# One block for attention and routing, with the weight fold laid out anew between logits, counts and lists

## The reference, cut to what matters

```python
for t in range(S):                                   # attention, r, k, v: (4, 8, 768, 48)
    cur = einsum('bhd,bhe->bhde', u * k_t, v_t)
    y[:, :, t] = einsum('bhd,bhde->bhe', r_t, state + cur)
    state = w * state + einsum('bhd,bhe->bhde', k_t, v_t)
...
do_compute = x @ w_skip > 0                          # experts, x: (3072, 384)
logits = xc @ w_gate; e_idx = argmax(logits, 1)      # w_gate: (384, 8)
gate_w = softmax(logits)[e_idx]
out = xc + gate_w * (relu(xc @ w1[e]) @ w2[e])       # w1: (8, 384, 1024), w2: (8, 1024, 384)
...
h = (x @ w1) * (x @ w2) @ w3                         # gated layers, w1, w2: (384, 1024), w3: (1024, 1024)
return h @ w_out                                     # w_out: (1024, 384)
```

## Time and profile before

| | us |
|---|---|
| median of 3 runs (lowest, highest) | 625.05 (624.2, 626.12) |
| profiled execution, its own time | 628.02 |
| its span | 626.2 |
| PE busy, sum over the span | 607.0 |
| DVE, ACT, POOL busy | 294.6, 225.7, 149.3 |

### The profile page before, as it was taken

One profiled execution on the slowest core, in us unless ns is written; L12 is line 12 of the kernel. 1 busy time (PEld: TensorE's weight loads), 2 busy tenths in 40 slices (PEclk: granted clock), 3 DMA queues, 4 the chain that ended last, 5 costly groups with the idle time before them and its releaser, 6 DMA issues. The chain is left out here.

```text
span 626.2 us, 17333 instructions
## 1 busy us (share of the span) xinstructions
PE 607.0 (97%) x7377; PEld 539.3 (86%) x7377; DVE 294.6 (47%) x456; ACT 225.7 (36%) x407; POOL 149.3 (24%) x183
## 2 busy tenths in 40 slices
PE   7799999899999999999999999999999999999997
PEld 7699999756899998999788888888898888888886
DVE  6468888286377787777021232132232224123222
ACT  2246556424455556563051132132222113123212
POOL 7467777234133433441150000000000000000000
PEclk9889999799999999999999999999999999999999
DMA  7668997785376565663220020020003001001001
GB/s 138 121 136 178 181 182 182 251 265 187 120 274 251 216 218 193 221 256 120 85 88 0 1 100 1 1 71 31 0 1 102 0 1 50 1 1 50 1 0 51
DMA packets 103673, 67.77 MB, mean 108 GB/s; under 512 B 79124, under 2 KB 97688, under 8 KB 103632
## 3 DMA queue, kind: packets, MB, share of 16 engines
q1 hardware_dynamic: 75696, 57.88, 30.5%
q10 hardware_dynamic: 26144, 4.74, 4.1%
q0 software_dynamic: 1792, 4.58, 1.9%
HBM read 55.92 MB, written 12.19 MB: 109 GB/s over the span
## 5 line engine op out<-in xcount | busy, mean ns | idle before, releaser
L1548 DVE TENSOR_TENSOR gl_g_sb<-gl_a_sb,gl_pab 128x512 f32<-128x512 f32 x48 | 33.0, 688 | 186.3 <-ACT gl_a_sb L1525 186.3
L1468 PE MATMUL gl_pab<-gl_xT_hi,wm_lo 128*128 128x512 f32 x288 | 112.9, 392 | 0.0
L1468 PE MATMUL gl_pab<-gl_xT_lo,wm_hi 128*128 128x512 f32 x288 | 112.8, 392 | 0.0
L1468 PE MATMUL gl_pab<-gl_xT_hi,wm_hi 128*128 128x512 f32 x288 | 112.1, 389 | 0.0
L1525 ACT ACTIVATE gl_a_sb<-gl_pab 128x512 f32<-128x512 f32 x48 | 28.8, 599 | 183.9 <-PE gl_pab L1468 183.9
L1468 PEld LDWEIGHTS gl_pab<-gl_xT_hi,wm_lo 128*128 128x128 f32 x288 | 54.0, 188 | 11.4
L1468 PEld LDWEIGHTS gl_pab<-gl_xT_hi,wm_hi 128*128 128x128 f32 x288 | 54.1, 188 | 10.6 <-DVE gl_xT_lo L1555 0.3
L1468 PEld LDWEIGHTS gl_pab<-gl_xT_lo,wm_hi 128*128 128x128 f32 x288 | 54.0, 188 | 10.5
L1234 PE MATMUL ex_ph<-ex_xT_hi,ew_w_hi 128*128 128x224 f32 x192 | 52.9, 275 | 0.0
L1234 PE MATMUL ex_ph<-ex_xT_hi,ew_w_lo 128*128 128x224 f32 x192 | 52.7, 274 | 0.0
L1234 PE MATMUL ex_ph<-ex_xT_lo,ew_w_hi 128*128 128x224 f32 x192 | 52.7, 274 | 0.0
(11 more groups left out here) (204 smaller groups left out, 1232.8 us busy)
## 6 DMA issues: line engine op xcount, KB each, us to landing
w_in<-in_moe_w SPq DMA_DIRECT2D x8, 1536.0 KB, 9.6
ew_w_in<-in_moe_w SPq DMA_DIRECT2D x8, 1536.0 KB, 6.5
w_in<-in_moe_w SPq DMA_DIRECT2D x14, 512.0 KB, 7.3
k_in<-in_k SPq DMA_DIRECT2D x48, 96.0 KB
v_in<-in_v ACTq DMA_DIRECT2D x48, 96.0 KB
r_in<-in_r SPq DMA_DIRECT2D x48, 96.0 KB
w_in<-xbuf SPq DMA_DIRECT2D x12, 384.0 KB, 4.1
out<-gl_o_sb SPq DMA_DIRECT2D x12, 384.0 KB, 2.4
```

The costliest lines, as they stand in the source:

```text
L1468: m = pe.matmul(p_ab[f % 2][w][:, :], a[:, w * KD + k, cols], b[t.slot][:, k, :], start=(k == 0 and n == 0), stop=(k == KD - 1 and n == 2))
L1548: dve.tensor_tensor(g_sb[f % 2][:, :], a_sb[f % 2][:, :], p_ab[f % 2][1][:, :], ALU.mult).then_inc(s_g, 1)
```

## The change

Attention and routing share one block, so the barrier between them is gone. Where routing's instructions read `lg` or load over memory that attention used, a new semaphore `s_logits`, raised by DVE's addition into `lg`, is waited for instead: by DVE before its first reduction, by POOL before `closed`, by SP before the load of `w1`. PE and ACT have no such wait.

The fold's pieces are laid out anew. With the whitespace of the changed indentation left out:

```diff
 # attention, SP
                     fold.load_w_out(sp)
-                    fold.load(sp, [1])
+                    fold.load(sp, [1, 2])
 ...
             sp.wait_ge(s_lg, 1)
-            fold.load(sp, [2])
+            fold.load(sp, [3])
             store_x(sp, env, xbuf, 1, 2, NCH - 2)
 # attention, PE
-                if f is logits and at(c, j, NT + 3):
-                    fold.turn(pe, 1, [p_R[:, i, :] for i in range(2)])
+                if f is logits and at(c, j, NT + 1):
                     fold.product(pe, 0, p_AU[:, 0, :], (0, 1))
+                if f is x_transposes and at(c, j, NT + 2):
+                    fold.turn(pe, 1, [p_R[:, i, :] for i in range(2)])
+                    fold.product(pe, 0, p_AU[:, 0, :], (2, 3))
 # attention, ACT
                 if f is y_out and at(c, j, NT + 2):
+                    fold.turned(act, 1, [p_R[:, i, :] for i in range(2)])
                     act.wait_ge(s_Y, BASE + NT + 1)
                     logits_out(NCH - 1).then_inc(s_lg, 1)
-                    fold.turned(act, 1, [p_R[:, i, :] for i in range(2)])
 # attention, DVE
-            dve.tensor_tensor(lg..., parts[:, 0], parts[:, 1], ALU.add)
+            dve.tensor_tensor(lg..., parts[:, 0], parts[:, 1], ALU.add).then_inc(env["s_logits"], 1)
 # routing, SP
-                fold.load(sp, [3])
                 fold.load(sp, [4])
+            sp.wait_ge(env["s_logits"], 1)
                 ex.load_w1(sp, 0)
 # routing, PE
-                fold.product(pe, 0, p_W[0], (2, 3))
                 fold.turn(pe, 2, p_T[0])
+            fold.product(pe, 1, p_W[1], (0, 1, 2))
                 pe.wait_ge(s_m, 2)
                 ... (the counts)
-                fold.product(pe, 1, p_W[1])
-                fold.product(pe, 2, p_W[0])
+            fold.product(pe, 1, p_W[1], (3,))
                 fold.turn(pe, 3, p_T[1])
+            fold.product(pe, 2, p_W[0])
+            fold.turn(pe, 4, p_T[0])
+            fold.product(pe, 3, p_W[1], (0, 1, 2))
                 ... (the first list)
-                fold.turn(pe, 4, p_T[0])
-                fold.product(pe, 3, p_W[1])
+            fold.product(pe, 3, p_W[1], (3,))
                 fold.turn(pe, 5, p_T[1])
 # routing, ACT: turned 3 ahead of the wait for s_slot, turned 4 ahead of the split of w1,
 #               taken 3 and turned 5 behind it
```

More of the change, by code:

```diff
@@ L111, in store_x, with attention @@
                      env["x_all"][pr][jj * HALF:(jj + 1) * HALF, 2 * c:2 * (c + chunks), :]).then_inc(env["s_stored"], 16)
-def attention(nc, env, r, k, v, w, u, xbuf):
+def attention(nc, env, sem, r, k, v, w, u, xbuf):
     B, H, S, D = r.shape
@@ L245, in half @@
             return slice(DP * i, DP * i + DP)
-        block = ctx.enter_context(nc.Block())
+        block = env["block"]
         @block.sync
@@ L425, in extra @@
                     fold.turn(pe, 0, [p_AU[:, i, :] for i in range(2)])
-                if f is logits and at(c, j, NT + 3):
+                if f is logits and at(c, j, NT + 1):
+                    fold.product(pe, 0, p_AU[:, 0, :], (0, 1))
+                if f is x_transposes and at(c, j, NT + 2):
                     fold.turn(pe, 1, [p_R[:, i, :] for i in range(2)])
-                    fold.product(pe, 0, p_AU[:, 0, :], (0, 1))
+                    fold.product(pe, 0, p_AU[:, 0, :], (2, 3))
             schedule(pe, ((turns_ready, 0), (k_transposes, 0), (x_transposes, -3), (r_transposes, 0), (natural, -2), (logits, -4), (inputs_ready, -1),
@@ new lines, in routing, with _, gate_step @@
+        block = env["block"]
+        @block.sync
+        def _(sp):
+            fold.load(sp, [4])
+            sp.wait_ge(env["s_logits"], 1)
+            ex.load_w1(sp, 0)
+            fold.load(sp, [5, 6])
+            ex.load_w2(sp, 0)
+            fold.load(sp, [7])
+        @block.gpsimd
+        def _(pool):
+            pool.wait_ge(env["s_logits"], 1)
+            pool.tensor_scalar(closed[:, :], lg[:, E, :], 0.0, 64.0, ALU.is_le, ALU.mult).then_inc(s_closed, 1)
+            for x in ex.x_in:
+                pool.memset(x[:, :, :], 0.0)
+            def gate_step(m):
+                n_gate[0] += 1
+                m.then_inc(s_gate, 1)
+                pool.wait_ge(s_gate, n_gate[0])
+            n_gate = [1]
+            pool.wait_ge(s_gate, 1)
+            gate_step(pool.tensor_copy(piece[:, 0, :], gate[:, :]))
+            gate_step(pool.tensor_tensor(rest[:, :], gate[:, :], piece[:, 0, :], ALU.subtract))
+            gate_step(pool.tensor_copy(piece[:, 1, :], rest[:, :]))
+            gate_step(pool.tensor_tensor(rest[:, :], rest[:, :], piece[:, 1, :], ALU.subtract))
+            gate_step(pool.tensor_copy(piece[:, 2, :], rest[:, :]))
+            pool.wait_ge(s_slot, 1)
+            slot_values(pool, 2, piece[:, 0, :], s_gval)
+            pool.wait_ge(s_table, 1)
+            pool.wait_ge(env["s_stored"], 32 * (NT // 4 + 2))
+            for i in range(2):
+                ex.gather(pool, xbuf, 0, i, env["slot_token"][0:ex.rows(i), i:i + 1])
+            for i in range(1, 3):
+                slot_values(pool, 2 + i, piece[:, i, :], s_gval)
+            pool.wait_ge(s_table, 3)
+            ex.take_gate(pool, env, 0, 0)
@@ new lines, in _ @@
+        @block.tensor
+        def _(pe):
+            fold.turn(pe, 2, p_T[0])
+            fold.product(pe, 1, p_W[1], (0, 1, 2))
+            pe.wait_ge(s_m, 2)
+            for p in (p_pos, p_slot):
+                pe.matmul(p, tb.before[:, :], mine, start=True, stop=False, skip_group_check=True)
+                m = pe.matmul(p, tb.ones[:, :], earlier[:, :], start=False, stop=(p is p_pos), skip_group_check=True)
+            pe.matmul(p_slot, tb.ones[0:1, :], tb.e_base[0:1, :, :].rearrange("p e t -> p (e t)"), start=False, stop=True, skip_group_check=True)
+            last = [x.rearrange("p (e t) -> p e t", t=NT)[:, :, NT - 1] for x in (mine, earlier[:, :])]
+            pe.matmul(p_tot, tb.ones[:, :], last[0], start=True, stop=False, skip_group_check=True)
+            pe.matmul(p_tot, tb.ones[:, :], last[1], start=False, stop=True, skip_group_check=True).then_inc(s_mm, 1)
+            fold.product(pe, 1, p_W[1], (3,))
+            fold.turn(pe, 3, p_T[1])
+            fold.product(pe, 2, p_W[0])
+            fold.turn(pe, 4, p_T[0])
+            fold.product(pe, 3, p_W[1], (0, 1, 2))
+            pe.wait_ge(s_near, 1)
+            for h in range(2):
+                pe.wait_ge(s_token, 2 + h)
+                for t in range(h * NT // 2, (h + 1) * NT // 2):
+                    m = pe.matmul(p_list[:, 0:2 * NSL], oh_lo[:, t, :], vals[:, t, 0:2, :].rearrange("p v s -> p (v s)"),
+                                  start=(t == 0), stop=(t == NT - 1))
+            m.then_inc(s_list, 1)
+            fold.product(pe, 3, p_W[1], (3,))
+            fold.turn(pe, 5, p_T[1])
+            fold.product(pe, 4, p_W[0])
+            fold.turn(pe, 6, p_T[0])
+            pe.wait_ge(s_table, 1)
+            pe.wait_ge(s_gval, 3)
+            for t in range(NT):
+                m = pe.matmul(p_list[:, 2 * NSL:5 * NSL], oh_lo[:, t, :], vals[:, t, 2:5, :].rearrange("p v s -> p (v s)"),
+                              start=(t == 0), stop=(t == NT - 1))
+            m.then_inc(s_list, 1)
+            fold.turn(pe, 7, p_T[1])
+            fold.product(pe, 5, p_W[1], (0, 1))
@@ new lines, in _ @@
+        @block.scalar
+        def _(act):
+            act.wait_ge(s_exp, 1)
+            act.activation(expo[:, :, :].rearrange("p e t -> p (e t)"), dif[:, :, :].rearrange("p e t -> p (e t)"), ACT.Exp).then_inc(s_exp, 1)
+            fold.taken(act, 0, p_W[0])
+            fold.turned(act, 2, p_T[0])
+            fold.taken(act, 1, p_W[1])
+            fold.turned(act, 3, p_T[1])
+            act.wait_ge(s_slot, 1)
+            act.activation(vals[:, :, 1, :], oh_hi[:, :, :], ACT.Copy, scale=tb.row[:, 0:1]).then_inc(s_near, 1)
+            fold.taken(act, 2, p_W[0])
+            fold.turned(act, 4, p_T[0])
+            ex.first_w1_hi(act)
+            fold.taken(act, 3, p_W[1])
+            fold.turned(act, 5, p_T[1])
+            fold.taken(act, 4, p_W[0])
+            for i in range(6, 8):
+                fold.turned(act, i, p_T[i % 2])
@@ L1594, in program @@
             "s_wmlo": sem("s_wmlo"), "lg": sb("lg", [P, E + 1, N // P]), "seq": S,
-            "s_stored": sem("s_stored"),
+            "s_stored": sem("s_stored"), "s_logits": sem("s_logits"),
             "slot_token": sb("slot_token", [P, NSL], I32),
@@ L1607, in program @@
         env["p_pair"] = c.enter_context(nc.psum_tensor("p_pair", [P, 2, 512], F32))
-        with ExitStack() as cx:
-            sbx, _ = scope(cx)
-            env["x_all"] = [sbx(f"x_all{i}", [P, S // (P // 2), DM]) for i in range(2)]
-            env["fold"].w3_in.append(sbx("w3_in2", [P, FM]))
-            attention(nc, env, r, k, v, w, u, xbuf)
-        for n in ("wm_hi", "wm_lo"):
-            env[n] = sb(n, [P, 2 * KD, FM], F32R)
-        w1_in = sb("w1_in", [P, KD, FM])
```

(18 more changed lines are left out.)

222 lines of the change are left out of this document (71 added, 151 removed).

## The result

The changed kernel takes 623.0 us in the median of 10 runs (621.02 to 624.43), the kernel before 625.52 in 10 runs on the same chips (623.29 to 627.18): a ratio of 0.996, 95% interval 0.9941 to 0.9979. It is faster by 2.5 us (1.3 to 3.7), half of the 4.9 forecast. A second comparison, of 12 runs with 35 of before, gave medians of 622.0 against 624.79, 2.8 us apart, and a ratio of 0.9949 (0.993 to 0.9967), which is 3.2 us (2.1 to 4.4). The time of 623.0 lies above the forecast's own range (619.0 to 622.0) and inside the wider one of 8 in 10 (618.9 to 623.3).

What follows compares the result with a forecast made beforehand. PE was taken as the bound, busy 607.0 of 626.2 us; its rearranged steps start the experts at 157.4 instead of 162.3, so 625.05 - 4.9 = 620.15, rounded 620.2 us; own range 619.0 to 622.0, 8 in 10 618.9 to 623.3.

Steps and rivals of the forecast that it cites:

- The sum on PE: Nine priced steps on PE from the tail of attention to the experts, starting at 157.4 instead of 162.3: 4.9 us gained.
- 5.4 us at most: Upper limit of the gain on PE between turn 0 and the experts: 3.2 us of slow clock plus 2.24 of gaps.
- the waits of 0.5 and 0.4: Waits expected on PE: 0.5 us before turn 4 for its load, 0.4 before the second list for POOL's values.
- Load 4: Weight load that PE needs for turn 4: landing at 137.6 by 3.57 MB at 274 GB/s, a wait of 0.5 us.
- The 134.2 by ring order alone: Landing of load 4 if it waited for its 2.62 MB alone: no wait on PE, kernel time 619.7 us.
- The step that failed: Carrying the 4.9 us gain from the profiled execution, 3.0 us above the median, to the median: 625.05 to 620.15 us.
- The 3.2 us of slow clock: Excess over full-clock price in attention's tail on PE: turn 1 0.86, half product 2.00, last logits 0.33 us.
- the 0.74 of "issue": Gap of 0.74 us on PE in the tail, released by issue, counted as hidden behind long matmuls after the change.
- The forecast without the clock's term: Gain if the clock falls in the tail all the same: 1.7 us, giving 623.4 us; chance 0.13.
- DVE's chain: Rival: `lg` or the one-hot tables 2 us late, first list and all behind 1.4 later, 621.6 us; chance 0.09.
- The queue: Rival: transfers at 200 GB/s make turn 4 wait 5.3 us and turn 5 0.3, 628.4 us; chance 0.05.
- The clock: Rival: PE's clock falls in the tail after the change too, losing 3.2 us, 623.4 us; chance 0.13.

Runs made afterwards that it cites:

- e7: The kernel before, unchanged, profiled one more time: 623.9 us in one run.
- e6: The kernel before, unchanged, profiled one more time: 626.46 us in one run.
- e1: The kernel before, unchanged, run and profiled again: 624.91 us in 12 runs against 624.79, ratio 1.0.
- e3: The changed kernel with the fold's pieces put back in the order of before, blocks still merged: 624.78 us in 12 runs, ratio 0.9988 to before.
- e4: The changed kernel with the second block and its barrier put back, new layout kept: 625.86 us in 12 runs, ratio 1.001 to before.
- e9: The merged block with the fold's pieces in the order of before, one more profile: 623.64 us in one run.
- e10: The merged block with the fold's pieces in the order of before, a third execution: 622.75 us in one run.
- e5: The kernel before with two groups of six dummy transposes in the tail's gaps on PE: 625.47 us in 12 runs against 625.92, ratio 0.9996.

## Where the prediction held and where it failed

**The sum on PE** (steps 1 to 9) held: it gave the experts' start as 157.4, measured 157.26 with turn 0 0.23 later. `lg` was ready at 125.6 (125.2 forecast, and 0.23 of that is the later start), the counts opened at 129.43 (129.1), the first list ran without a wait, the second waited for POOL, 0.23 for my 0.4. The "5.4 us at most" was too low: 4.9 and the waits of 0.5 and 0.4 in the same sum make 5.8, and the stretch between these two profiles shrank by 5.26 with waits of 0.1 and 0.23 left.

**Load 4** landed at 137.6, the very number of the estimate from bytes moved. A part of that is luck: load 3 was issued 0.4 us later than in my sum, and 3.46 MB had moved by the landing instead of 3.57. The 134.2 by ring order alone was wrong: 0.84 MB of later transfers had moved before load 4 was complete. The term was still too large: PE, 0.3 us later than in my sum, met it with a wait of 0.1 instead of 0.5. The Trainium skill's page "DMA: Bandwidth & Descriptors", section "Queues, rings and completion order", says that completion is not first in, first out; the 0.84 MB agree.

**The step that failed** is the last of the sum: "the sum is made against that execution, which is 3.0 us above the median (0.5%), and I carry the same difference over". The 3.2 us of slow clock in that sum, and the 0.74 of "issue", are not a cost of before's median but of one kind of its executions, the costliest of the four that were profiled. Four profiles of before lose 3.75, 2.24, 1.95 and 0 us in this stretch against the clean course, 2.0 on average; the change saves 1.6 us in a clean execution, and whatever the clock takes in one that is not. That makes 1.6 to 5.3, with 3.6 as the mean over these four; measured were 2.5 and, by the ratio of the second comparison, 3.2, and 3.6 lies inside both intervals. The forecast without the clock's term, 4.9 - 3.2 = 1.7, is within 0.1 us of what executions without the hole show (43.94 - 42.35), but by luck: two errors of 0.5 cancel. The sum has 44.5 for that stretch of before, with the "issue" gap in it that e7 lacks, and 42.8 for after, with 0.6 more of waits than were measured. I had the 1.7, but only as a rival, in which the clock falls *after* the change; that it might not fall *before* it was not among the cases. The sign was there to read: the profiled execution lay 3.0 us over the median, and the slow clock's term was 3.2. That the two are so close is no measure of the term: e6 lay 0.5 over its median and lost 1.95.

**The rivals.** DVE's chain did not become the bound. The queue did not starve turns 4 and 5, though turn 4 waited 0.1 us for its load in the first profile. The clock did not fall in the tail in the two profiles of after.

Shown by runs: that the hole comes and goes in one unchanged program (e1, e6, e7); that merge and layout are worth little or nothing apart (e3, e4, e9, e10); that with the gaps filled the low mean clocks are gone (e5). Still open: what decides in which execution the clock falls, and why the "issue" gap ranges from none to 0.74 us. With the tail as in before and no dummies, both profiles without that gap kept the clock (e7, e9), and of the five with it four lost it (the first, e1, e3, e6) and one did not (e10, 0.46 us), so the gap may belong to the cause or to the effect. Open too is how often before's executions have the hole: 3.6 is a mean of four profiles, and part of its difference from the measured 2.5 can be chance.

## What to carry to other kernels

Before a term of slow clock goes into a sum, ask whether the median pays it: hold the profiled execution's own time and mean clock against the other runs, and where it lies above them by about that term, forecast with a share of the term, or take more profiles. When a barrier goes, ask which work stood behind it on the bounding engine; here it paid more than 0.5 us only because the work that everyone waited for could then be put behind work that filled the gaps. And a barrier also waits for the engine that issues transfers (e4).

## What the hardware showed that I had not expected

- PE's clock fell from 2.4 to 1.2 GHz in three of four profiles of one program, after gaps of 0.61, 0.21 and 0.19 to 0.74 us between small matmuls, at moments that differed by up to 1.8 us counted from turn 0. Each fall cost 1.8 to 3.0 us. In e1 and e6 it came about 0.9 us after turn 1 had begun, with PE busy since then. In a single idle stretch of 2.88 us (e4) it fell just before 126 and stayed at half until after 132.
- SP's issue of load 4 took 2.64 us and that of `w1` 2.23 us with three earlier transfers outstanding each time, against 0.33 for load 3 with none:

```profile
125.02 0.33 SPq L61 DMA_DIRECT2D w_in<-in_moe_w  x1
125.40 1.25 SPq L110 DMA_DIRECT2D xbuf<-x_all  x2
126.69 2.64 SPq L61 DMA_DIRECT2D w_in<-in_moe_w  x1
129.37 2.23 SPq L998 DMA_DIRECT2D w_in<-in_moe_w  x1
```

No engine in this kernel waited for it.
